# Two U/V loads on the SyncE queue moved 34 slots earlier, and one VectorE mix placed ahead of a softmax normalisation

## The reference

```
attention:  scores = q k^T / 8 ; heads 0-3 see the last 32 tokens,
            heads 4-7 every 4th of the last 128 ; softmax (sum + 1e-9) ; times v
x = heads joined                                          (B, S, 512)
channel mix: x_prev = x shifted by one token
            xk = mu_k x + (1 - mu_k) x_prev ; xr = mu_r x + (1 - mu_r) x_prev
            x = sigmoid(xr w_r) * (relu(xk w_k)^2 w_v)    w_k: 512 x 1024
token mix:  u = x + ((x^T U) V)^T                         U: 576 x 32, V: 32 x 576
out = u + relu(u w_ch1) w_ch2                             w_ch1: 512 x 2048
```

## Time and profile before

| | |
|---|---|
| median of 3 runs | 754.3 us |
| profiled execution | 754.3 us, its span 752.5 us |
| TensorE busy in the span | 728.3 us (97%), 4860 matmuls |
| VectorE, ScalarE, GpSimd busy | 328.2, 302.2, 166.8 us |
| mean granted clock | 0.999 of 2.4 GHz |

### The profile page before, as it was taken

One profiled execution on the slowest core, in us unless ns is written; L12 is line 12 of the kernel. 1 busy time (PEld: TensorE's weight loads), 2 busy tenths in 40 slices (PEclk: granted clock), 3 DMA queues, 4 the chain that ended last, 5 costly groups with the idle time before them and its releaser, 6 DMA issues.

```text
span 752.5 us, 13122 instructions
## 1 busy us (share of the span) xinstructions
PE 728.3 (97%) x4860; PEld 638.1 (85%) x4860; DVE 328.2 (44%) x687; ACT 302.2 (40%) x814; POOL 166.8 (22%) x257
## 2 busy tenths in 40 slices
PE   4899999999999999999999999999999999999998
PEld 3677878988888887888898999999899999999997
DVE  5788886777677535725222221312221131213111
ACT  4687867777768656734331111211111111111110
POOL 6998121202122151415770000000000000000000
PEclk9999999999999999999999999999999999999999
DMA  7876454545533320002440102101010210111001
GB/s 143 186 183 122 105 133 95 102 103 127 104 89 101 87 63 29 29 8 87 155 115 13 43 1 43 42 0 26 16 42 0 42 42 0 18 24 43 0 1 43
DMA packets 165843, 49.00 MB, mean 65 GB/s; under 512 B 142880, under 2 KB 159776, under 8 KB 165792
## 3 DMA queue, kind: packets, MB, share of 16 engines
q1 hardware_dynamic: 129088, 43.99, 23.4%
q10 hardware_dynamic: 36704, 4.34, 3.8%
HBM read 34.98 MB, written 9.37 MB: 59 GB/s over the span
## 4 chain that ended last, share of the span: by engine, by line
PE 85%; SPq 5%; DVE 3%; DMA 2%; ACT 2%; issue 1%; ACTq 1%; POOL 0%; DVEq 0%
PE bank L1383 27%; PE bank L1385 26%; PE bank L1384 26%; SPq L524 2%; PE bank L1441 2%; PE bank L1404 2%; SPq L628 1%; ACT probs L830 1%; DMA probs_dram<-probs_blocks 1%; PE bank L1532 1%; SPq L551 1%; ACTq L840 1%; DMA probs_t<-probs_dram 1%; PE bank L1544 1%; SPq L537 1%
## 5 line engine op out<-in xcount | busy, mean ns | idle before, releaser
L1350 DVE SCALAR_TENSOR_TENSOR h_l<-bank,h_h 128x384 fp32r<-128x384 f32 x96 | 53.5, 557 | 289.6 <-ACT h_h L1076 289.6
L1076 ACT ACTIVATE h_h<-bank 128x384 fp32r<-128x384 f32 x96 | 47.2, 491 | 317.6 <-PE bank L1385 317.6
L1385 PE MATMUL bank<-ut_h,w_l 128*128 128x384 f32 x384 | 129.4, 337 | 0.0
L1383 PE MATMUL bank<-ut_h,w_h 128*128 128x384 f32 x384 | 129.3, 337 | 0.0
L1384 PE MATMUL bank<-ut_l,w_h 128*128 128x384 f32 x384 | 128.9, 336 | 0.0
L1385 PE MATMUL bank<-w_h,h_l 128*128 128x512 f32 x288 | 113.7, 395 | 0.0
L1384 PE MATMUL bank<-w_l,h_h 128*128 128x512 f32 x288 | 113.5, 394 | 0.0
L1383 PE MATMUL bank<-w_h,h_h 128*128 128x512 f32 x288 | 112.0, 389 | 0.0
L1383 PE MATMUL bank<-xs_h,wk_h 128*128 128x256 f32 x288 | 83.9, 291 | 0.3
L1384 PE MATMUL bank<-xs_l,wk_h 128*128 128x256 f32 x288 | 81.3, 282 | 0.0
L1385 PE MATMUL bank<-xs_h,wk_l 128*128 128x256 f32 x288 | 81.2, 282 | 0.0
(11 more groups left out here) (123 smaller groups left out, 1159.8 us busy)
## 6 DMA issues: line engine op xcount, KB each, us to landing
stage<-in_moe_w_ch_dram SPq DMA_DIRECT2D x16, 512.0 KB, 3.4
out_dram<-result SPq DMA_DIRECT2D x18, 256.0 KB, 2.1
u_tile<-result SPq DMA_DIRECT2D x80, 48.0 KB, 2.0
probs_dram<-probs_blocks SPq DMA_DIRECT2D x12, 240.0 KB, 2.1
probs_t<-probs_dram SPq DMA_DIRECT2D x36, 80.0 KB, 2.2
k_raw<-in_k_dram ACTq DMA_DIRECT2D x64, 40.0 KB, 2.3
q_raw<-in_q_dram SPq DMA_DIRECT2D x64, 40.0 KB, 2.2
q_raw<-in_q_dram SPq DMA_DIRECT2D x64, 32.0 KB, 2.1
```

The costliest lines, as they stand in the source:

```text
L1076: act.activation(h_h[:, m % KRING, :], h_bank[m % 2][:, 0:C2], ACT.Relu).then_inc(hh_done, 1)
L1350: dve.scalar_tensor_tensor(h_l[:, m % KRING, :], h_bank[m % 2][:, 0:C2], 0.0, h_h[:, m % KRING, :].bitcast(F32), op0=ALU.max, op1=ALU.subt ...
L1383: pe.matmul(dst, lhs[0], rhs[0], start=start, stop=False)
L1385: return pe.matmul(dst, lhs[1], rhs[0], start=False, stop=stop)
```

## The change

Two edits. The loads of U and V move from the end of slot 60 to the end of slot 26 of the SP queue (`2 * NUNIT + UNIT["k", 4]` is 20 + 6). And VectorE does the mixes of a slot ahead of `normalise` and `turn_probs` of the same slot. Nothing is added or removed.

```diff
@@ the SP queue's loop over slots @@
                 for n in [nth(k, p) + VALUES for k, p in pairs_in("D", slot - 1)]:
                     if nth(2, 0) <= n < NPART * PAIRS:
                         load_v(*divmod(n, PAIRS))
-                if slot == (NPART - 2) * NUNIT:
+                if slot == 2 * NUNIT + UNIT["k", 4]:
                     load_u()
                     load_piece(PIECE_V)
@@ VectorE, chunk(c) @@
                     if n >= 1 and UNITS[n - 1][0] == "k":
                         square(c, UNITS[n - 1][1])
+                    for t in range(KT):
+                        if not last and n == MIX_SLOT[c][t]:
+                            mix(c + 1, t)
                     for k, p in pairs_in("T", slot + n):
                         normalise(k, p)
                         turn_probs(k, p)
-                    for t in range(KT):
-                        if not last and n == MIX_SLOT[c][t]:
-                            mix(c + 1, t)
```

## The result

The changed kernel takes 761.55 us in the median of 8 runs (758.17 to 763.27), the kernel before 755.1 us (753.34 to 756.43). The ratio is 1.008 with a 95% interval of 1.0058 to 1.0101. That is 6.4 us more. The forecast was 3.2 us more, 757.5 us, with a range up to 759.0; direction and place were right, the size was not.

The account below looks back on a forecast made before the run. The prediction took TensorE's stream to bound the kernel, with the SP queue nearly as critical at chunk borders. It summed 754.3 + 3.2 (stall at D(4,1)) + 0 + 0 = 757.5 us, range 755.6 to 759.0.

Parts of the forecast that it names:

- The block takes 4.24 us of the queue, its own waits hold nothing: SP queue, slot 26: the eight U and V DMAs occupy it 4.24 us; only their issuing counts.
- The margin is 0.7 us at D(4,1), and the stall is 3.2 us: At D(4,1), the 4.2 us block exceeds the 0.7 us margin; TensorE idles 3.2 us more, 2.7 to 3.5.
- my two conditions for from_dram(4,1): SP queue: it must get there, 147.03 or 146.2 us, and to_dram(4,1) must have landed, 146.7 us, taken as likeliest.
- Rival (c): Slow issue leaves D(5,1)'s run, 756.4 us, or falls ahead of from_dram(4,1), 758.3; or chunk 1's 0.7 us unabsorbed, 758.2; 18%.
- The sum: an idle microsecond of TensorE costs a microsecond: Whole kernel: the 3.2 us stall at D(4,1) was added in full to 754.3 us, giving 757.5 us.
- Not given back later; D(5,1) keeps its wait: TensorE behind D(4,1): everything moves by the 3.2 us stall, and the 1.12 us wait ahead of D(5,1) stays.
- Nothing gained at slot 60: SP queue where the U and V loads leave: at most 0.2 us of queue, no TensorE wait, taken as 0.
- The mix order: net 0 by repayment at D(3,1): Chunk 1's end: TensorE waits 0.6 us more, then less at D(3,1); taken as 0, bounds -0.2 to +0.7 us.
- the wait for `xs_l` at 108 us: Sign of being right, on TensorE at the next chunk's first matmul: a wait of 0.6 us.
- (a): Slot 26: the insertion is hidden, its eight DMAs taking under 0.7 us of queue; time stays 754.3 us; chance 12%.
- (b): Issue hiccups come by DMA count; one leaves D(5,1)'s queue run, its 1.12 us wait vanishes; 753.2 us; chance 3%.
- (d): Extra transfers crowd the DMA engines, delaying both landings of (4,1) by 1 us each; 759.5 us; chance 5%.

Follow-up runs that it names:

- fills: Changed kernel plus matmuls with overwritten results ahead of probs-transfer waits: 24 at D(4,1), 761.31 us; with 9 each at D(3,1) and D(5,1) too, 760.59 us.
- the tiny DMAs: Kernel before, U and V still at slot 60, plus eight DMAs of 16 KB in all in slot 26: 760.54 us, ratio 1.0067.
- the single fill: Changed kernel plus 24 matmuls with overwritten results on TensorE ahead of D(4,1)'s wait for the probs transfer: 761.31 us, ratio 1.0078.

## Why the prediction was wrong, point by point

- *What bounds the kernel.* Right: TensorE's stream, and the SP queue at the chunk borders.
- *The block takes 4.24 us of the queue, its own waits hold nothing.* Right: 4.28 us.
- *The margin is 0.7 us at D(4,1), and the stall is 3.2 us.* The margin held. The stall was 4.05 us, 0.85 more than forecast, and 3.05 and 3.2 in two further profiles, of the changed kernel and of the loads alone. Of my two conditions for from_dram(4,1) the wrong one was named: to_dram(4,1) landed in 1.8 us, not 2.9, and the queue itself was last (1.8 is also below the estimate of 2.3 from the Trainium skill, whose section is on DMAs issued by GpSimd, where SyncE issues this one). And an issue took 1.46 us more than its like where I had carried over 0.8. Rival (c) had this term with its size; I gave it its own case instead of letting it widen the forecast's. With this error alone the time would have been 758.35 us, inside the range. The prediction also read the issues as 0.43 to 0.65 us each all through the queue; the earlier trace rows have them from 0.34 to 1.17.
- *The sum: an idle microsecond of TensorE costs a microsecond.* This step failed, and it was never written down as a step. The low clock behind the wait cost 2.81 us, nearly as much as the stall was to cost. The prediction says nothing of the clock behind the stall, which puts this term at nothing without a reason; in the earlier trace rows waits of 1.57 and 1.12 us stood without a fall of the clock, but the new wait was to be twice as long. The page "TensorE: Matmul & The Clock Gate" of the Trainium skill, section "HAM oscillation — how this bites in real kernels", says that a wait for DMA, if long enough, makes the engine's clock be throttled again, so that the work behind starts slow. The runs agree: 0.50 behind all four waits at D(4,1) of 2.65 us and more without fills (3.96, 3.2, 3.05 and 2.65). The 6.8 us of low clock in this one profile are the long case; behind the other three waits it was 3.4 us. The one execution of the changed kernel at a mean clock of 1.0 took 758.72 us, inside the range.
- *Not given back later; D(5,1) keeps its wait.* The first half is right: +6.9 us from chunk 3 on, 7.0 at the end. The second is wrong for the profiled execution: D(5,1) waited 0.57 instead of 1.12 us, and with D(3,1), 1.09 instead of 1.57, the sum of the two changed, which the prediction had named as a sign of being wrong. It brought no time, since chunk 3's 6.9 us stood unchanged behind chunk 6.
- *Nothing gained at slot 60.* Right: no difference arises there.
- *The mix order: net 0 by repayment at D(3,1).* Right, and shown by itself. In the changed kernel's own profile the wait for `xs_l` at 108 us, named as a sign, doesn't stand.
- *Rivals.* (a) fell with the result, and the tiny DMAs show why: it is the sequencer's time, and 0.5 us of it is not small beside a transfer of 2.2. (b) didn't happen. (d) fell with the same run: 4% of the bytes, the same loss.

With the 4.05 and 2.81 us in place of 3.2 and 0, the sum is 754.3 + 6.9 = 761.2 us, beside 761.35 of the profiled execution.

## What to carry to other kernels

A queue that issues DMAs is an engine with a sum of its own, some 0.5 us for each DMA here and not by its size: 0.43 us for one of 2 KB, 0.60 for one of 24 KB, 0.37 for one of 512 KB. Before anything is put into it, find the transfer behind it that has least to spare, and price the block as its length less that margin. Then price the wait as its length plus the stretch at the low clock that may follow it. Behind 100 us, no wait of up to 1.85 us in these profiles was followed by one; of six waits from 1.90 to 2.26 us four were, each by 3.4 us; and so were all four from 2.65 us on, by 3.4 us and in one case 6.8. These are counts from the profiles of this kernel, not a rule. The wait's length alone doesn't decide it: in the start-up of the kernel before, the clock stayed at 1.00 behind waits of 5.76 and 2.03 us.

## What the runs showed of the hardware that I had not expected

Some DMA issues take 1 to 2 us instead of 0.45. In the changed kernel's q load of (5,3) one of the four did:

```profile
L524 SPq DMA_DIRECT2D q_raw<-in_q_dram x4: 422/462/1945, 139.0 to 141.9; - x4
```

They coincide with packets of the queue that carries instructions (q8). In the kernel before, seven of its packets fall between 98 and 184 us, and exactly seven issues of the SP queue took more than 0.8 us there, each starting within 0.5 us of one of them (98.9, 114.0, 128.7, 140.0, 153.9, 166.3 and 182.9 us). There is one in the 0.3 us from 139.2 of the changed kernel, ahead of this slow issue, one at 139.6 to 140.2 in the kernel before, where q of (6,0) was slow, and one at 182.3 to 183.3 with the single fill, where from_dram(5,1) took 2.92 instead of 1.37 us before and made D(5,1) wait 2.26. The rows, in that order:

```profile
q8 instruction: 1, 0.02, 33.4%
```

```profile
q8 instruction: 1, 0.02, 9.8%
```

```profile
q8 instruction: 1, 0.02, 8.2%
```

They don't come by the number of DMAs, as rival (b) supposed, but at nearly the same times with 8 DMAs more in the queue: between 128 and 129 us in both kernels, and next at 139.2 to 139.5 in the one, 139.6 to 140.2 in the other. The page "Runtime: NRT & Kernel Launch" of the Trainium skill, section "Instruction fetch mechanics", says that each sequencer drives a DMA queue of its own to fetch the next block of instructions, and that this is hidden by the pace of issue. The first half fits. That the fetch causes the slow issue is inferred from the coincidence; no experiment took it away. If it does, it is not hidden in a queue without slack: the slow issue ahead of from_dram(4,1) stood in the changed kernel's stall.
